# Attention encoder with two MLPs: tile 0's inverse diagonal by blocks, its x split over two banks and two engines, its first exponentials in halves, and its last score chunks before tile 1's

## The reference

```
kv_pool = kv.reshape(B, H//4, 4, W//4, 4, C).mean(axis=(2, 4))
k = v = kv_pool.reshape(B, -1, C) @ w_sr
s = (q @ k.transpose(0, 2, 1)) / sqrt(C)
a = exp(s - s.max(-1)); a /= a.sum(-1) + 1e-9
x = a @ v
h = x @ moe_w_in                       # first MLP
g = where(h >= 1, h, where(h <= -1, 0, (h + 1)**2 / 4))
y = g @ moe_w_out
h = y @ moe2_w_in                      # second MLP
out = (h * sigmoid(1.702 * h)) @ moe2_w_out
```

## Time and profile before

| | us |
|---|---|
| median of 3 runs | 1293.2 |
| lowest, highest | 1292.01, 1294.04 |
| profiled execution | 1293.84 |
| its span | 1292.0 |
| PE busy | 1274.2 (99%) |
| POOL busy | 1144.8 (89%) |
| ACT busy | 1005.7 (78%) |
| DVE busy | 992.5 (77%) |

### The profile page before, as it was taken

The page is one execution under the profiler, slowest core; times in us unless marked ns, Lnnn a source line. Parts: engine busy times, 40 slices in busy tenths (PEclk is TensorE's granted clock), DMA queues, the critical chain, the costliest instruction groups (busy, mean ns, idle before and its releaser), DMA issues.

```text
span 1292.0 us, 17064 instructions
## 1 busy us (share of the span) xinstructions
PE 1274.2 (99%) x5518; PEld 1028.3 (80%) x5518; DVE 992.5 (77%) x1138; ACT 1005.7 (78%) x1070; POOL 1144.8 (89%) x491
## 2 busy tenths in 40 slices
PE   8999999999999999999999999999999999999998
PEld 5656888888888888888888888888888888888876
DVE  6778977878779788787797887877978878776443
ACT  3686887787888878887878788878787888797666
POOL 5738999999999999999999999999999999979780
PEclk9999999999999999999999999999999999999999
DMA  9100100000000000000000000000000000000000
GB/s 346 38 25 8 34 17 17 17 18 33 16 16 33 16 16 16 16 33 16 16 26 19 20 16 16 33 16 17 19 17 28 16 17 25 9 17 18 1 9 17
DMA packets 18259, 35.74 MB, mean 28 GB/s; under 512 B 3248, under 2 KB 3376, under 8 KB 17968
## 3 DMA queue, kind: packets, MB, share of 16 engines
q1 hardware_dynamic: 18224, 35.30, 8.2%
HBM read 28.90 MB, written 6.39 MB: 27 GB/s over the span
## 4 chain that ended last, share of the span: by engine, by line
PE 88%; POOL 4%; DVE 3%; issue 2%; ACT 2%; DMA 1%; SPq 0%; POOLq 0%; ACTq 0%; DVEq 0%
PE ps_ring L505 17%; PE ps_ring L507 16%; PE ps_ring L506 16%; PE ps_y L505 12%; PE ps_y L507 12%; PE ps_y L506 12%; POOL g_lo L411 3%; PE ps_y L661 1%; DVE s_sb L1086 1%; DMA q_sb<-in_q_t 1%; ACT g L929 0%; ACT g L924 0%; PE ps_y L620 0%; DVE g L1145 0%; PE ps_ring L532 0%
## 5 line engine op out<-in xcount | busy, mean ns | idle before, releaser
L411 POOL TENSOR_TENSOR g_lo<-g,g_hi 128x1024 fp32r<-128x1024 f32 x363 | 922.8, 2572 | 73.0 <-DVE g L1145 63.2
L1136 DVE SCALAR_TENSOR_TENSOR g_hi<-g,ps_ring 128x1024 fp32r<-128x1024 f32 x182 | 221.7, 1218 | 141.7 <-ACT g L929 141.5
L910 ACT ACTIVATE g<-ps_ring 128x1024 f32<-128x1024 f32 x192 | 197.2, 1027 | 168.2 <-PE ps_ring L507 167.9
L505 PE MATMUL ps_y<-g_hi,w_hi 128*128 128x512 f32 x748 | 294.5, 394 | 3.2 <-POOL g_lo L411 1.9
L507 PE MATMUL ps_y<-g_hi,w_lo 128*128 128x512 f32 x748 | 291.2, 389 | 0.0
L506 PE MATMUL ps_y<-g_lo,w_hi 128*128 128x512 f32 x748 | 291.1, 389 | 0.0
L1145 DVE SCALAR_TENSOR_TENSOR g<-g,ps_ring 128x1024 f32<-128x1024 f32 x192 | 233.0, 1214 | 5.3 <-ACT g L929 5.2
L929 ACT ACTIVATE g<-g 128x1024 f32<-128x1024 f32 x192 | 204.2, 1063 | 5.4
L924 ACT ACTIVATE g<-ps_ring 128x1024 f32<-128x1024 f32 x192 | 198.0, 1031 | 7.7 <-PE ps_y L661 6.4
L912 ACT ACTIVATE g_hi<-ps_ring 128x1024 fp32r<-128x1024 f32 x192 | 195.9, 1020 | 6.2 <-PE ps_y L507 6.2
L505 PEld LDWEIGHTS ps_y<-g_hi,w_hi 128*128 128x128 f32 x748 | 140.4, 188 | 40.5 <-POOL g_lo L411 9.6
(11 more groups left out here) (139 smaller groups left out, 1697.4 us busy)
## 6 DMA issues: line engine op xcount, KB each, us to landing
kv_sb<-in_kv_t SPq DMA_DIRECT2D x12, 512.0 KB, 9.0
q_sb<-in_q_t SPq DMA_DIRECT2D x24, 256.0 KB, 3.6
out_t<-y_sb SPq DMA_DIRECT2D x24, 256.0 KB, 3.5
key_max<-max_row SPq DMA_DIRECT2D x23, 256.0 KB, 3.3
inv_sum<-inv_row SPq DMA_DIRECT2D x23, 256.0 KB, 3.2
w_raw<-in_moe_w_in SPq DMA_DIRECT2D x2, 1024.0 KB, 16.9
max_row<-max_turned SPq DMA_DIRECT2D x23, 2.0 KB, 1.3
inv_row<-inv_turned SPq DMA_DIRECT2D x23, 2.0 KB, 1.3
```

The costliest lines, as they stand in the source:

```text
L411: return nc.gpsimd.tensor_tensor(dst, src, upper.bitcast(F32), ALU.subtract)
L505: nc.tensor.matmul(dst, l_hi, r_hi, start=start, stop=False)
L910: nc.scalar.activation(g2[:, slot, :], ps_h2(it, k), ACT.Gelu_apprx_sigmoid).then_inc(g2_done, 1)
L1136: nc.vector.scalar_tensor_tensor(out=g1_hi[:, uu % 2, :], in0=g1[:, uu % 2, :], scalar=1.0, in1=ps_h1(it, k), op0=ALU.min, op1=ALU.max).th ...
```

## The change

Four edits, all for tile 0:

- PE computes the last two score chunks of tile 0 before chunk 3 of tile 1.
- ACT takes the exponential of the first pair in two halves, each with a semaphore; PE releases them chunk by chunk, and starts values of chunk 0 after the first half. The upper half of tile 2's q comes behind the exponentials.
- The diagonal of inverses is made in four blocks of 128 columns with `tensor_scalar`, each with an increment of `inverse_masked`; PE waits for them one by one. POOL's wait for `inverse_masked >= 1` stays as it is.
- x lands in two PSUM banks (`ps_two`), two blocks in each. DVE makes upper and lower part of the first half, ACT the upper part of the second half, DVE its lower part. ACT's copy stands before its evictions of tile 2.

```diff
+        def ps_x_turned(half):
+            return ps_two[:, half, 0:2 * P]
...
-                    if c % 2 == 1:
+                    if c < 2:
+                        last.then_inc(chunk_subtracted, 1)
+                    elif c % 2 == 1:
                         last.then_inc(max_subtracted, 1)
...
+                    pe.wait_ge(exp_half, 1)
+                elif c == 1:
+                    pe.wait_ge(exp_done, 1)
+                elif c % 2 == 0:
...
-                pe.wait_ge(inverse_masked, 1)
                 for b in range(QUADS):
-                    last = nc.tensor.matmul(ps_y1[:, b * P:(b + 1) * P], o_t[:, b, :], inv_diag[:, b, :], start=True,
-                                            stop=True)
-                last.then_inc(x_turned, 1)
+                    pe.wait_ge(inverse_masked, b + 1)
+                    last = nc.tensor.matmul(ps_x_turned(b // 2)[:, (b % 2) * P:(b % 2 + 1) * P], o_t[:, b, :],
+                                            inv_diag[:, b, :], start=True, stop=True)
+                    if b % 2 == 1:
+                        last.then_inc(x_turned, 1)
...
                 pe.wait_ge(x_hi_done, t + 1)
+                if t == 0:
+                    pe.wait_ge(x_hi_half, 1)
...
                 pe.wait_ge(x_lo_done, t + 1)
+                if t == 0:
+                    pe.wait_ge(x_lo_half, 1)
...
-            whole_scores(1, 3)
             whole_scores(0, 4)
             whole_scores(0, 5)
+            whole_scores(1, 3)
...
+            def exponential_first_half(c):
+                act.wait_ge(chunk_subtracted, c + 1)
+                nc.scalar.activation(s_sb[:, 0, c, :], ps_s(0, c), ACT.Exp).then_inc(exp_half if c == 0 else exp_done, 1)
+
             def exponential_first(p):
-                act.wait_ge(max_subtracted, p + 1)
+                act.wait_ge(max_subtracted, p)
...
+            exponential_first_half(0)
+            exponential_first_half(1)
+            for p in range(1, PAIRS):
+                exponential_first(p)
             act.wait_ge(q_loaded[2], 16)
             copy(q2_hi[:, :], q2_sb[:, :]).then_inc(q_hi_done, 1)
-            for p in range(PAIRS):
-                exponential_first(p)
             act.wait_ge(v_copied, 2)
             copy(v_hi[:, :, :], v_sb[:, :, 0:C]).then_inc(v_hi_done, 1)
             o_copy()
+            act.wait_ge(x_turned, 2)
+            copy(x_hi[:, 0, 2 * P:T], ps_x_turned(1)).then_inc(x_hi_done, 1)
...
-                nc.vector.tensor_tensor(inv_diag[:, :, :], ident[:, :].unsqueeze(1).to_broadcast([P, QUADS, P]),
-                                        inv_first[:, :].unsqueeze(2).to_broadcast([P, QUADS, P]),
-                                        ALU.mult).then_inc(inverse_masked, 1)
+                for b in range(QUADS):
+                    nc.vector.tensor_scalar(inv_diag[:, b, :], ident[:, :], inv_first[:, b:b + 1], None,
+                                            ALU.mult).then_inc(inverse_masked, 1)
 
             def split_first():
                 dve.wait_ge(x_turned, 1)
-                nc.vector.tensor_copy(x_hi[:, 0, :], ps_y1[:, :]).then_inc(x_hi_done, 1)
+                nc.vector.tensor_copy(x_hi[:, 0, 0:2 * P], ps_x_turned(0)).then_inc(x_hi_half, 1)
+                dve.wait_ge(x_hi_half, 1)
+                lower(x_lo[:, 0, 0:2 * P], ps_x_turned(0), x_hi[:, 0, 0:2 * P]).then_inc(x_lo_half, 1)
                 dve.wait_ge(x_hi_done, 1)
-                lower(x_lo[:, 0, :], ps_y1[:, :], x_hi[:, 0, :]).then_inc(x_lo_done, 1)
+                lower(x_lo[:, 0, 2 * P:T], ps_x_turned(1), x_hi[:, 0, 2 * P:T]).then_inc(x_lo_done, 1)
```

More of the change, by code:

```diff
@@ L214, in encoder_kernel @@
         max_masked = sem("max_masked")
+        chunk_subtracted = sem("chunk_subtracted")
         max_subtracted = sem("max_subtracted")
@@ L221, in encoder_kernel @@
         x_turned = sem("x_turned")
+        x_hi_half = sem("x_hi_half")
+        x_lo_half = sem("x_lo_half")
+        exp_half = sem("exp_half")
         shifted = sem("shifted")
@@ L591, in first_values @@
                     pe.wait_ge(k_copied, 2)
-                if c % 2 == 0:
+                    pe.wait_ge(exp_half, 1)
+                elif c == 1:
+                    pe.wait_ge(exp_done, 1)
+                elif c % 2 == 0:
                     pe.wait_ge(exp_done, c // 2 + 1)
```

## The result

| | before | after |
|---|---|---|
| median, us (20 runs each) | 1293.43 | 1295.85 |
| lowest, highest | 1291.78, 1297.8 | 1293.73, 1297.43 |
| profiled execution, its span | 1293.84, 1292.0 | 1295.5, 1293.7 |
| PE resumes at line 661 (after: 678) | 43.76 | 45.27 |
| first shift of tile 1, start and end | 39.46, 41.36 | 39.94, 42.87 |

What follows compares the result with a forecast made beforehand. Transfers of max_row and key_max, then the first shift, were taken to bound the opening; gains end waiting there, PE resuming at 43.8 against 43.76: change 0.0, forecast 1293.2 us, range 1291.6 to 1296.3.

Steps and rivals of the forecast that it cites:

- rival B: Opening: GpSimd's next w_lo slips ahead of the first shift; PE resumes 1.7 to 1.9 us later, 1295.0; chance 0.20.
- C: Opening: rival B or the stalls, plus a fall of PE's clock; +3.4 us on top of B, 1296.6; chance 0.12.
- the stall of the blocks: Inverse diagonal: one block held 2.37 us by GpSimd's w_lo, last block behind it, block 3 ending at 37.75.
- the place of the shift: Tile 1's first shift: follows GpSimd's casts, ahead of its next w_lo, from 39.75 to 40.9 instead of ending 41.36.
- What bounds the opening: Before line 661: g waits on max_row and key_max transfers, max_row landing behind queued loads at 36.1 regardless.
- the 39.44 taken as fixed: Landing of key_max, which releases tile 1's first shift: claimed unmoved by the change, within 0.2 us.
- Score order, exponentials, blocks, x: The edits' own effects: project_v and copies 0.62 us later, values 0.36 sooner, blocks 0.29 at most, x halves 0.42.
- the pair at 102.40: Two later shifts, 4.53 us with a whole g_lo between: read as whole-instruction exclusion, the waiting one getting the next turn.
- 35.16 as the point: GpSimd's w_lo start: if earlier than this, its next w_lo precedes the shift; estimated start 35.2.
- D: Later pair of shifts: both go before g_lo, removing 2.4 us idle and a 1.6 us clock loss; about 1289; chance 0.06.

Runs made afterwards that it cites:

- run 3: Changed kernel with the inverse diagonal made by one 512-column tensor_tensor as before, all other parts kept: 1293.66 us, ratio to before 1.0000.
- run 4: Changed kernel, but GpSimd starts w_lo of the third matrix only after the first shift is done: 1295.66 us, ratio to before 1.0022.
- run 9: Changed kernel, GpSimd waiting for all blocks, fourth weights and tile 3's queries loaded behind tile 1's maxima, tile 3's third shift behind two evictions: 1290.19 us.
- run 11: Changed kernel with GpSimd waiting for all four blocks and tile 3's third shift moved behind two evictions of tile 4: 1291.45 us, ratio 0.9987.
- run 5: Kernel before, with the load of tile 3's queries issued behind the two transfers of tile 1's maxima: 1292.97 us, ratio 0.9994.
- run 6: Changed kernel, GpSimd waiting for all four blocks, fourth weight matrix and tile 3's queries issued behind tile 1's maxima: 1292.67 us, ratio 0.9997.
- run 1: Changed kernel, but GpSimd waits for all four blocks of the inverse diagonal instead of the first: 1293.85 us, ratio to before 1.0000.
- run 8: Changed kernel with nothing altered, profiled once more in its slowest group of times: 1296.18 us.
- run 10: Changed kernel with only tile 3's third shift moved behind two evictions of tile 4: 1294.34 us, ratio to before 1.0007.
- run 2: Kernel before with only the inverse diagonal split into four tensor_scalar blocks, GpSimd released by the first: 1298.57 us, ratio 1.0038.

## Why the prediction was wrong

The time, 1295.85, lies in the range; the forecast of no change and its sum were wrong, and the case that came was rival B with part of C, at a chance of 0.20 and 0.12. Two steps of the sum failed, the stall of the blocks and the place of the shift; runs 3 and 4 show that either one alone makes PE late.

- *What bounds the opening: right.* Runs 9 and 11 show it: with max_row not behind the loads, PE resumes 1.24 us sooner, and with it behind them the change has nothing to gain. The one row given for it was read loosely: the transfers' share of 0.04 is that of the stretch from 34 to 36, before the two landings at 35.93 and 36.11, and does not show that max_row waited for the loads; runs 5 and 6 do. key_max was issued at 36.14 and took 3.4 us, so it landed near 39.5, against the 39.44 taken as fixed; in other executions it came up to 0.9 later (40.33 in run 1), where the prediction allowed 0.2.
- *Score order, exponentials, blocks, x: right in size.* project_v(1) 25.88 (26.0 forecast), ScalarE's copies 0.52 later (0.62), values 28.70 (28.77), a block 0.28 (0.29 at most), GpSimd's w_lo at 35.11 (35.2).
- *What GpSimd does to the blocks: the mechanism right, its term mis-sized.* This is the first step that failed. The forecast took "one stall of 2.37, with the last block behind it", block 3 done at 37.75. Measured were two holds, 2.39 and 1.06: GpSimd, released at 35.02, asks before the third block does, and its cast is already waiting when that block is through. The last block ended at 38.51, 0.76 later, and x_lo at 39.93 instead of 38.9. Run 4 prices the late x: 1.0 us. The turn-taking read from the pair at 102.40 said this; I applied it once and not to the instruction that GpSimd has queued behind. The two holds stood only in rival B. The Trainium skill (SBUF — State Buffer, section "Who interferes with whom") has tensor_scalar among the instructions that can take the shared pair; this case agrees: 0.28 us with GpSimd out of the way (run 1), 2.39 with its w_lo running.
- *The shift against GpSimd's series: the wrong side of a close point.* This is the second step that failed: the sum has the shift run from 39.75 to 40.9, ahead of the next w_lo. I named 35.16 as the point and put GpSimd at 35.2 to 35.3. It started at 35.11, its next w_lo at 39.38, and x_lo ended at 39.93. With x that late the shift came behind w_lo wherever key_max landed; and as key_max landed near 39.5, also behind 39.38, an x in time would not have saved it. The shift ended at 42.87. The margin (35.11 against 35.16) lies within what single executions differ by, so on which side of it an execution falls is partly luck. B's figures, PE at 45.4 to 45.7 and 1295.0, stand against 45.27 and 1295.85.
- *The clock: underrated.* C put a fall in the opening at 0.12. Of the four profiled executions in which the changed kernel's blocks were held (the first profile, runs 4, 8 and 10), two had it (8 and 10), and run 2 had it as well. In the profiles PE resumes 1.5 us later without it and 2.1 with it (run 8, 45.82). The mean clocks say how often it came: ten of the 20 executions of the changed kernel have 0.997 or less, the value with two falls, and two of before's 87. At equal falls the change costs 1.9 us (1.000) and 1.4 us (0.998 and 0.999), near the 1.5 of the profiles, and a second fall puts half of its executions 1.6 us higher. That closes the sum to a few tenths; why it is 1.9 where nothing falls stays open.
- *D: the mechanism was read right and priced too high.* Taking the pair apart gave 1.85 us, not 4: g_lo came last in its place, so only 0.65 us of the idle time went, and the rest is the clock.

## What to carry to other kernels

A semaphore that is raised earlier also releases whoever else waits for it: before splitting an instruction into blocks, look for every waiter, and ask what the engine that starts sooner will contend for with the blocks that are still to come. Where two engines take turns on a resource, lay out the queue of both behind the first collision, not only the instruction at hand. And a stage that already waits for a transfer can't be made faster by its compute; move what is queued ahead of the transfer.

## What the runs showed of the hardware

- VectorE's tensor_scalar of f32 from SBUF to SBUF takes turns with GpSimd's two-input and casting instructions: 0.28 us alone, 2.39 behind w_lo, 1.06 behind a cast. With both engines loaded the turns alternated, one block to one GpSimd instruction.
- A transfer of 2 KB took 1.35 us with an empty queue ahead of it (run 6), 3.48 behind a weight matrix (run 5), 4.27 behind that and a load of queries (before), each from its issue to the issue of the transfer that waits for it.
- The granted clock fell in some executions and not in others behind the same idle of PE. Run 4 had PE busy 0.13 of 2 us from 108 to 110 and kept 1.00 from 110 to 116; the changed kernel, with the same gap (0.00 of 2 us), had 0.50 from 112 to 114. The kernel before had a mean clock of 1.000 in 30 of 87 executions and less in the others, 1.6 us apart.
- A race decided by 0.01 us (run 3) cost 2.3 us of shift. That kernel's times spread from 1291.04 to 1297.76; how much of this is the race and how much the clock was not told apart.
